# Four weight sums on GpSimd, and the last result's steps ahead of the block adds, at the border of two layers

## The reference

```python
scores = cap * tanh(scale * q @ k.T / cap)
attn = softmax(scores) @ v                      # x: 896 x 768
h = x @ w_in                                     # layer 1
g = where(h > 0, h, exp(min(h, 0)) - 1)
x = g @ w_out
h = x @ w_in2                                    # layer 2
g = maximum(0.01 * h, h)
return g @ w_out2
```

## Time and profile before

| what | value |
| --- | --- |
| median of 3 runs | 575.67 us (574.37 to 577.39) |
| the profiled execution's own time | 574.71 us |
| its span | 572.9 us |
| TensorE busy | 556.7 us, 97% |
| VectorE busy | 469.4 us, 82% |
| ScalarE busy | 352.8 us, 62% |
| GpSimd busy | 275.2 us, 48% |
| granted TensorE clock | 1.000 |

### The profile page before, as it was taken

One profiled execution on the slowest core, in us unless ns is written; L12 is line 12 of the kernel. 1 busy time (PEld: TensorE's weight loads), 2 busy tenths in 40 slices (PEclk: granted clock), 3 DMA queues, 4 the chain that ended last, 5 costly groups with the idle time before them and its releaser, 6 DMA issues.

```text
span 572.9 us, 8610 instructions
## 1 busy us (share of the span) xinstructions
PE 556.7 (97%) x2908; PEld 499.4 (87%) x2908; DVE 469.4 (82%) x758; ACT 352.8 (62%) x606; POOL 275.2 (48%) x273
## 2 busy tenths in 40 slices
PE   6999989999999999999999999989999999999997
PEld 5777779889998999999999999879999998999997
DVE  5899998878875133898988999889999779999881
ACT  6999988999995455654644454536454445544440
POOL 6779998799965655552000003856666530000000
DMA  6455564455423333335644332031113225536251
GB/s 174 106 143 128 150 174 125 123 130 146 98 65 89 98 112 110 111 108 165 213 135 158 131 99 67 1 110 56 57 55 90 77 84 192 159 119 220 84 170 51
DMA packets 34172, 67.07 MB, mean 117 GB/s; under 512 B 6864, under 2 KB 18768, under 8 KB 34128
## 3 DMA queue, kind: packets, MB, share of 16 engines
q1 hardware_dynamic: 33984, 66.28, 39.4%
q10 hardware_dynamic: 144, 0.23, 0.1%
HBM read 63.70 MB, written 2.80 MB: 116 GB/s over the span
## 4 chain that ended last, share of the span: by engine, by line
PE 77%; DVE 10%; ACT 4%; issue 3%; POOL 3%; DMA 2%; ACTq 0%; SPq 0%; DVEq 0%; POOLq 0%
PE mlp_ps L1129 8%; PE mlp_ps L1131 8%; PE mlp_ps L1130 8%; PE o_ps L1129 6%; PE o_ps L1131 6%; PE o_ps L1130 6%; PE scores L1129 4%; PE scores L1130 4%; PE scores L1131 4%; PE probs_t L1103 4%; PE probs_t L1131 4%; PE probs_t L1130 4%; PE probs_t L1129 4%; PE scores L1088 2%; PE o_ps L1122 2%
## 5 line engine op out<-in xcount | busy, mean ns | idle before, releaser
L559 POOL TENSOR_TENSOR w_lo<-w_raw,w_hi 128x768 fp32r<-128x768 f32 (+1 forms) x62 | 104.2, 1681 | 62.3 <-ACT w_hi L621 61.9
L559 POOL TENSOR_TENSOR w_lo<-s_sum,w_hi 128x384 fp32r<-128x384 f32 x32 | 38.8, 1228 | 114.5 <-ACT w_hi L621 114.5
L621 ACT ACTIVATE w_hi<-s_sum 128x768 fp32r<-128x768 f32 (+1 forms) x64 | 43.4, 684 | 76.6 <-DVE s_sum L880 51.9
L621 ACT ACTIVATE w_hi<-w_raw 128x768 fp32r<-128x768 f32 (+1 forms) x77 | 56.5, 737 | 31.1 <-PE o_ps L1131 15.7
L601 ACT ACTIVATE soft<-soft,neg_max 112x448 f32<-112x448 f32 x96 | 63.6, 673 | 1.8 <-DVE soft L758 1.7
L758 DVE TENSOR_SCALAR_CACHE_REDUCE soft<-soft,neg_abs 112x448 f32<-112x448 f32 x96 | 60.9, 671 | 2.2 <-ACT soft L591 1.9
L1129 PE MATMUL mlp_ps<-x_hi,w_hi 128*128 128x448 f32 x132 | 49.2, 373 | 0.4 <-issue 0.4
L765 DVE TENSOR_TENSOR p_lo<-probs_t,p_hi 112x896 fp32r<-112x896 f32 x37 | 40.3, 1089 | 10.0 <-ACT p_hi L610 9.9
L1130 PE MATMUL mlp_ps<-x_lo,w_hi 128*128 128x448 f32 x132 | 48.2, 365 | 0.0
L1131 PE MATMUL mlp_ps<-x_hi,w_lo 128*128 128x448 f32 x132 | 48.2, 365 | 0.0
L591 ACT ACTIVATE soft<-scores 112x896 f32<-112x896 f32 x47 | 43.4, 924 | 6.0 <-PE scores L1089 5.9
(11 more groups left out here) (238 smaller groups left out, 1747.7 us busy)
## 6 DMA issues: line engine op xcount, KB each, us to landing
w_raw<-w_units SPq DMA_DIRECT2D x120, 384.0 KB, 3.2
q_raw<-qT SPq DMA_DIRECT2D x24, 224.0 KB, 3.1
k_raw<-kT SPq DMA_DIRECT2D x23, 224.0 KB, 3.0
v_raw<-v_rows SPq DMA_DIRECT2D x24, 112.0 KB, 3.2
inv_all<-inv_rows SPq DMA_DIRECT2D x24, 112.0 KB, 3.4
y_t<-y_out SPq DMA_DIRECT2D x12, 224.0 KB, 2.8
inv_rows<-row_inv SPq DMA_DIRECT2D x24, 1.8 KB, 3.1
k_raw<-kT ACTq DMA_DIRECT2D x1, 224.0 KB, 3.1
```

The source lines that it names most:

```text
L559: pool.tensor_tensor(w_part(w_lo, n), w_source(n), f32(w_part(w_hi, n)), ALU.subtract).then_inc(w_lo_pool, 1)
L621: nc.scalar.activation(w_part(w_hi, n), w_source(n), ACT.Copy).then_inc(w_hi_done, 1)
```

## The change

GpSimd forms the four weight sums of block 0, by a new function `first_block_sum` with a semaphore of its own, ahead of its low parts for the blocks. VectorE no longer forms them. Behind `second(0)` its queue is reordered: `x_low("p1")`, y12 and y11 come first, then the sums of block 1 and the low parts of p5 and p6 in turn, then `add_to` for the last result y21, and directly behind it `x_low("p2")` and the fourth difference, which were in the loop. ScalarE's `x_high("p2")` moves ahead of its loop, that is ahead of high parts 8 and 9 and `block_keep(0)`.

```diff
@@ -154,7 +154,7 @@
 LO_ON_POOL = [n for n in range(ITEMS) if n not in LO_ON_DVE]
 
 SUM_ITEMS = ([n for n in range(GEMM1) if item_name(n)[1] in SUMS]
-             + [GEMM1 + BLOCK_AT[i, p] for i in range(HF) for p in SUMS]
+             + [GEMM1 + BLOCK_AT[i, p] for i in range(1, HF) for p in SUMS]
              + [n for n in range(GEMM2[1], ITEMS) if item_name(n)[1] in SUMS])
 X_GROUPS = ("p3", "p7", "p1", "p5", "p6", "p2", "p4")
 
@@ -314,7 +314,7 @@
         w_lo_pool, w_lo_dve = sem("w_lo_pool"), sem("w_lo_dve")
         unit_done, pair_done, tail_done = sem("unit_done"), sem("pair_done"), sem("tail_done")
         relu_done, act_done, g_done = sem("relu_done"), sem("act_done"), sem("g_done")
-        s_done = sem("s_done")
+        s_done, s_pool_done = sem("s_done"), sem("s_pool_done")
         t1_done, t2_done, t3_done, t4_done = (sem(f"t{i}_done") for i in range(1, 5))
         g_hi_done, g_split = sem("g_hi_done"), sem("g_split")
         p1_kept, u2_done, u4_done, u3_done = sem("p1_kept"), sem("u2_done"), sem("u4_done"), sem("u3_done")
@@ -370,6 +370,8 @@
             return w_lo_pool, LO_ON_POOL.index(n) + 1
 
         def sum_done(n):
+            if item_name(n)[0] == "blocks" and item_name(n)[2] == 0:
+                return s_pool_done, SUMS.index(item_name(n)[1]) + 1
             return s_done, SUM_ITEMS.index(n) + 1
 
         def loaded(r):
@@ -558,6 +560,28 @@
                 pool.wait_ge(*high_done(n))
                 pool.tensor_tensor(w_part(w_lo, n), w_source(n), f32(w_part(w_hi, n)), ALU.subtract).then_inc(w_lo_pool, 1)
 
+            def first_block_sum(p):
+                n = GEMM1 + BLOCK_AT[0, p]
+                raws = ITEM_RAWS[n]
+                for r in raws:
+                    pool.wait_ge(*loaded(r))
+                pool.wait_ge(*split_done(GEMM1 - 9))
+                dst, (lo, hi) = w_source(n), (slice(0, HALF), slice(HALF, UNIT))
+                if p == "p6" or p == "p3":
+                    ahead = GEMM1 + BLOCK_AT[0, SUMS[SUMS.index(p) - 1]]
+                    pool.wait_ge(*sum_done(ahead))
+                    before = w_source(ahead)
+                a11, a12 = w_raw[:, raws[0] % RAW, lo], w_raw[:, raws[0] % RAW, hi]
+                if p == "p5":
+                    args = a11, a12, ALU.add
+                elif p == "p7":
+                    args = a11, w_raw[:, raws[1] % RAW, lo], ALU.subtract
+                elif p == "p6":
+                    args = before, a11, ALU.subtract
+                else:
+                    args = a12, before, ALU.subtract
+                pool.tensor_tensor(dst, *args).then_inc(s_pool_done, 1)
+
             pool.memset(zero[:, :], 0.0).then_inc(zero_set, 1)
             pool.memset(ident[:, :], 0.0).then_inc(ident_set, 1)
             pool.wait_ge(ident_set, 1)
@@ -578,6 +602,9 @@
                 if s in (13, 17, 21):
                     split_w((s - 13) // 4)
             for n in LO_ON_POOL[units_ending_at(STEPS - 1)[0] + AHEAD:]:
+                if n == GEMM1:
+                    for p in SUMS:
+                        first_block_sum(p)
                 split_w(n)
 
         @block.scalar
@@ -722,13 +749,12 @@
             x_high("p6")
             w_high(GEMM1 + 6)
             w_high(GEMM1 + 7)
+            x_high("p2")
             for q in range(GEMM1 + 1, GEMM2[1]):
 
                 i, p = BLOCK_SEQ[q - GEMM1 - 1]
                 if p == "p1" and i != 1:
                     block_keep(i)
-                if i == 0 and p == "p1":
-                    x_high("p2")
                 if i == 0 and p == "p6":
                     leak(0, "p3")
                 if i == 1 and p == "p1":
@@ -1007,26 +1034,25 @@
                 if f in (11, 13, 15):
                     second_sum(0, (f - 11) // 2)
             second(0)
-            for p in SUMS:
-                weight_sum(GEMM1 + BLOCK_AT[0, p])
-
-            weight_sum(GEMM1 + BLOCK_AT[1, "p5"])
-            weight_sum(GEMM1 + BLOCK_AT[1, "p6"])
             x_low("p1")
             dve.wait_ge(xc_split, X_GROUPS.index("p1") + 1)
             x_sum(y12, y12, y11, ALU.subtract)
+            x_sum(y11, y22, y11, ALU.add)
+
+            weight_sum(GEMM1 + BLOCK_AT[1, "p5"])
+            x_low("p5")
+            weight_sum(GEMM1 + BLOCK_AT[1, "p6"])
+            x_low("p6")
             weight_sum(GEMM1 + BLOCK_AT[1, "p3"])
-            x_low("p5")
-            x_sum(y11, y22, y11, ALU.add)
             weight_sum(GEMM1 + BLOCK_AT[1, "p7"])
-            x_low("p6")
             dve.wait_ge(u3_done, HC)
             add_to(0, "p4", y21, kept_u2[0], y21_done)
+            x_low("p2")
+            dve.wait_ge(xc_split, X_GROUPS.index("p2") + 1)
+            x_sum(y21, y21, y11, ALU.subtract)
             for q in range(GEMM1 + 1, GEMM2[1] + 1):
 
                 i, p = BLOCK_SEQ[q - GEMM1 - 1]
-                if i == 0 and p == "p6":
-                    x_low("p2")
                 if p == "p6":
                     block_add(i, "p6")
                 if i == 0 and p == "p6":
@@ -1034,8 +1060,6 @@
                     block_add(0, "p7")
                     block_hidden(0, "p3")
                     block_hidden(0, "p7")
-                    dve.wait_ge(xc_split, X_GROUPS.index("p2") + 1)
-                    x_sum(y21, y21, y11, ALU.subtract)
                 if i == 1 and p == "p5":
                     x_low("p4")
                 if i and p in ("p3", "p7") or p in ("p2", "p4"):
```

## The result

The changed kernel takes 577.77 us (median of 20 runs), the kernel before 574.69 in the same comparison (20 runs): ratio 1.0057, 95% interval 1.0046 to 1.0067, so 3.3 us slower. The forecast was 2.4 us slower. The clocks of the records matter here: of the 20 executions of the changed kernel 17 show a mean granted TensorE clock of 0.997 or less; of 72 of the kernel before, timed beside the experiments, 5 do. The mean doesn't say where in the kernel the clock was lower; for that the windows of a trace are read.

A forecast was written before the change was run, and what follows sets the result against it. TensorE was taken as the bound, with 2.4 us of border gaps to win. (1, p3) 2.9 us later less 0.5 for a closed gap gave +2.4 on the median of 575.67: 578.1, range 574.7 to 581.0.

The forecast's parts named there:

- own signs of being wrong: VectorE idling or GpSimd missing its turn between 351 and 369, or TensorE's step after (1, p3) not being 0.205.
- What bounds the kernel: TensorE, busy 97% of the span; only its gaps in the border, 2.4 us, can be won by this change.
- The sums' price: Each block 0 sum on GpSimd: 0.87 us in turn, 0.97 alone, as for split_w; range 0.5 to 1.8.
- full turn: Each GpSimd TENSOR_TENSOR in flight beside VectorE's instructions with two SBUF inputs costs VectorE 0.87 us; beside PSUM reads, nothing.
- VectorE's queue up to y21: From 351.3, 11.0 us of VectorE work plus 7.0 of GpSimd turns; the adds for y21 start at 369.3.
- The new gap at (1, p1): TensorE before (1, p1): waits for y21_done, ready at 370.9 but due at 369.7; a new gap of 1.3 us.
- The fourth difference's end: VectorE's fourth data difference, now ahead of the block adds, ends at 376.1, after the low part and GpSimd's turn.
- (1, p3) at 379.9: TensorE starts (1, p3) at 379.9, after block adds delayed by the fourth difference: 2.9 us later than 377.03.
- The gaps at (0, p6) and (0, p4): TensorE's first and third border gaps, 0.4 and 0.5 us, close because x_low of p6 and p4 are ready in time.
- rival B: TensorE's clock falls in the longer gap at (1, p3): 1.9 us more, +4.3 in all, 580.0; chance 0.12.
- Rival A: GpSimd's turns cost VectorE little, all border gaps close: 2.4 us faster, 573.3; chance 0.15.
- Rival C: A sum on GpSimd is dearer than a low part: at 1.3 us each about +4.1, 579.8; chance 0.13.

The follow-up runs named there:

- experiment 7: Changed kernel with fourth difference back behind the block adds, two block 1 sums and block 0's first block add in VectorE's wait, block_keep(0) earlier: 572.04 us, ratio 0.9957.
- Experiment 1: Changed kernel with one step undone: the fourth data difference stands again behind the two block_hidden of block 0; 574.05 us, ratio 0.9993 to the kernel before.
- experiment 4: Changed kernel with sixteen small transposes on TensorE between (1, p6) and (1, p3), filling part of the gap; 576.02 us, ratio 1.0039 to the kernel before.
- experiment 5: Changed kernel in which GpSimd forms weight low parts 3 to 6 of the border twice; 579.69 us, ratio 1.0087 to the kernel before.
- experiment 2: Kernel before with only the four sums of block 0 moved to GpSimd, nothing reordered; 574.77 us, ratio 1.0007.
- experiments 6: Changed kernel with fourth difference back behind the block adds, and sums of (1, p3) and (1, p7) moved behind the adds into y21; 572.70 us, ratio 0.9969.
- only-order kernel: Changed kernel with the four sums back on VectorE, so only the order of the queues differs from the kernel before; 579.28 us, ratio 1.0073.
- second run: The kernel of experiment 7 timed once more, unchanged; 572.13 us, ratio 0.9960 to the kernel before.

## Why the prediction came out as it did

**The time: near the forecast, and partly by luck.** 578.1 was forecast and 577.77 measured, but the 578.1 stands on a median of 575.67 from three runs, where twenty give 574.69. The change itself was forecast at +2.4 and measured at +3.3 (2.6 to 3.9). Two of the prediction's own signs of being wrong came: VectorE idled between 351 and 369, and TensorE's step after (1, p3) was for a while 0.37 and not 0.205.

**What bounds the kernel: right.** Gains and losses came through TensorE, by its gaps and, against the text, its clock behind one of them; the bound of 2.4 us on what can be won is about what experiment 7 reached (2.5 and 2.3 by the ratios).

**The sums' price: right but for the first.** Alone a sum took 1.02, as taken from `split_w` (0.97), and the two that met VectorE's low part and g_low cost these 0.4 and 0.8 us, within the 0.87 of a full turn. The first took 3.80, not 0.87 to 1.8: sum p7 came 2.1 us later than walked (352.93 + 0.43 against 351.3), `x_high("p1")` at 353.8 in place of 351.8, and VectorE did idle, 2.68 us, where the text said never.

**VectorE's queue up to y21: the number right by luck, by errors that cancel.** 369.3 forecast, 368.92 + 0.43 = 369.35 measured. The walk began at 351.3, 2.0 us late, since the first two sums were to take turns from VectorE; they took none, and the weight low part began at 348.87 + 0.43 = 349.30. Turns cost 6.2 us (1.2 for the later sums, 5.0 for low parts) and not 7.0: GpSimd did two low parts in VectorE's idle time, and 5.7 turns were paid behind it, not 8. Against these 2.8 us stand the 2.7 of idle time that the walk didn't have.

**The new gap at (1, p1), 1.3 forecast: 1.33. The fourth difference's end at 376.1: 376.3. (1, p3) at 379.9: 379.95, a gap of 3.3: 3.30.** The gaps at (0, p6) and (0, p4) closed as said. Experiment 1 shows that the difference ahead of the block adds is the cause.

**The clock: the term that the sum lacked.** The sum held nothing for it; rival B stood beside it with a chance of 0.12 and a price of 1.9. It came on top of the forecast, at 1.56 us in the trace; a mean clock of 0.997 or less stands with 17 of 20 executions, against 5 of 72 of the kernel before. With it the sum is 4.0, against 3.3 measured (2.6 to 3.9): 0.1 us beyond the interval. Why is not shown; the two steps of the last section can hide as much. The reason given against it was only that no gap of the trace before was as long. The Trainium skill (TensorE: Matmul & The Clock Gate, section Why this matters for your kernels) names idle gaps of this kind as what returns the engine to its lower clock; experiment 4 agrees, by 1.00 in place of 0.66 with half of the gap filled.

**Rival A (turns cost little) is refuted** by the turns in the traces of the changed kernel and of experiment 5. **Rival C (a sum is dearer)** holds for the first sum, but not for the time: experiment 2 costs 0.4 us.

## What to carry to other kernels

When a stage is moved ahead in one engine's queue, ask what it now stands in front of, and who waits for that: here a difference that only the fourth product after needed was put ahead of the adds that empty the next bank. The places for moved work are the engine's own waits (here for ScalarE's copy); in experiments 6 and 7 it cost TensorE nothing there. And an idle time of TensorE that grows longer than any in the trace has to be priced twice, by its length and by the clock behind it: here 3.1 us brought the lower clock, and 1.6 did not.

## What was not expected of the hardware

TensorE's step between matmuls has two values at a granted clock of 1.00, and mostly changes at a restart. The windows from 440 to 460 us of the kernel before and of the changed one:

```profile
440.00:460.00 20.00, 20.00 (x98) 18.17 (x97) 15.27 (x24) 9.06 (x18) 11.40 (x10) 1.00 0.27 79
```

```profile
440.00:460.00 20.00, 20.00 (x100) 18.55 (x99) 17.09 (x27) 10.61 (x21) 11.26 (x11) 1.00 0.26 78
```

98 matmuls against 100 in the same 20 us, with the engine never idle. From the starts in the timelines the step is 0.2067 us (438 steps from 383.54 to 474.06) against 0.2027 (450 steps from 384.65 to 475.85). In the kernel before the longer step begins with the restart at 383.05 and ends with a short wait at 474.4, some 90 us or 1.8 us lost; in the changed kernel this stretch has the shorter step. In the only-order kernel the longer step lasts from 385 to the end. Which of the two follows a restart differs between executions of one program. Experiment 7 and its second run are the same kernel, and the same window of the two traces shows 101 and 98 matmuls:

```profile
440.00:460.00 20.00, 20.00 (x101) 18.52 (x100) 16.32 (x24) 8.14 (x15) 11.05 (x9) 1.00 0.33 100
```

```profile
440.00:460.00 20.00, 20.00 (x98) 18.17 (x97) 15.29 (x23) 8.84 (x16) 11.12 (x9) 1.00 0.31 97
```

Their spans are 569.9 and 571.8 us. The second has the longer step for some 107 us more than the first (375.7 to 471.8 above all), which makes 2.1 us and so the whole difference of 1.9. In the first it also changed once without a restart: 0.2067 up to 380.5, 0.2027 behind it, in a row of matmuls without a gap. How much of the scatter of some 4 us between the other executions it makes is not shown. It also hides in a pair of traces: the spans before and after the change differ by 2.9 us, while the border's gaps and the clock alone would make 4.0. What sets it was not tried.
